# Calls within an attention head in another order on TensorE, ScalarE and VectorE

## The chip, the cores and the metric

The kernel runs on one core of one Trainium2 chip. The metric is the device time of one execution in microseconds (us). The kernel before takes a median of 836.47 us over 3 runs, between 835.2 and 836.91. TensorE (PE), VectorE (DVE), ScalarE (ACT) and GpSimd (POOL) each work through a queue of their own in program order; SyncE (SP) issues nearly all DMAs. They meet only through semaphores.

## What is computed

Attention in which a query sees only the keys of its own cluster, then two feed-forward layers, all in float32:

```python
# q, k, v: (2, 8, 768, 64); centroids: (8, 16, 64)
q_assign = argmax(q_n @ c_n.T); k_assign = argmax(k_n @ c_n.T)
scores = where(q_assign[:, None] == k_assign[None, :], q @ k.T / 8, -1e9)
attn = exp(scores - max(scores)); attn /= sum(attn) + 1e-9
x = reshape(attn @ v)                        # (1536, 512)
h = x @ w_in                                 # 512 -> 2048
x = where(h >= 1, h, where(h <= -1, 0, (h + 1) ** 2 / 4)) @ w_out
xn = x / rms(x) * rms_g
out = (silu(xn @ w_gate) * (xn @ w_val)) @ w_out2     # 512 -> 1536 -> 512
```

## The kernel before, in words

**The two stages.** Batch times heads gives 16 heads (`NH`), numbered 0 to 15. The attention of all heads fills roughly the first 286 us; the feed-forward layers follow, in 60 steps of products (`up`, L730, and `down`, L768). Every float32 operand is split in a high and a low part, so that a product is made of two or three products of parts. The first `up` waits for the last head's reciprocals (`reciprocals_copied`, L734).

**Blocks.** `blocks` (L291) calls a function `blk` of each engine for n = -3 to 16. Blocks -3 to 3 and 10 to 16 are written out (`fixed` is the number), blocks 4 to 9 are a loop over pairs of an even (u = 0) and an odd block (`fixed` is None). In block n the engines do, for four different heads at once:

- the probabilities and the output of head n ("pt"), with the last two output products of head n - 1;
- scores and exp of head n + 1, tiles 1 to 5, and tile 0 of head n + 2 (`scored`, L301);
- the mask of head n + 2 ("msk"), and the cluster products and the loading of q and k of head n + 3 ("asg", "t").

`on` and `present` leave out what lies outside heads 0 to 15. So block 14 has no loading, mask or cluster work, and block 16 only the end of head 15.

**The calls.** With the numbers that the prediction uses:

- `scores(t)` (PE, L585; called "scores t"): four products into the PSUM pair `ps_s`. There is one such pair, so it waits until `cut(t)` (DVE, L1317) of the tile before has read it. `cut` copies the tile to `sf` and takes its minimum; `exp(t)` (ACT, L869) makes probabilities in `pbuf` and their sum. `sf` has two buffers. Scores 5 begins a new head and waits for its q and k (`qk_assembled`).
- `probs_t(j)` (PE, L618, "probs j"), j = 0 to 8: four transposes of probabilities into one of four PSUM banks (`USES`, L242, gives each use its bank; `slot_free`, L265, waits for its last reader). `high(j)` (ACT, L861) and `low(j)` (DVE, L1327) split the bank into `pth` and `ptl`, three buffers each, and `pv(j)` (PE, L631, "pv j") multiplies these with the values `vs` into `ps_o`. Probs 0 of a head waits for all of its exps.
- `output` (ACT, L885) copies `ps_o` to `osb` after pv 8. SP moves half of it to the other partitions (`moved`, L510), POOL adds it (`tpair`, L2001).
- `transpose_qk` (PE, L648), `qk_high` (ACT, L897) and `qk_low` (DVE, L1361) load and split q and k; SP copies them in place (L496 to L499).
- `assign` (PE, L658), `assigned` and `hits` (DVE, L1369 and L1379), the rank product `eqr` (POOL, L2026), `masks` (DVE, L1346, two compares into `mskin`), `mask_t` (PE, L677, into `ps_o`, so it waits for `output`), `masks` (ACT, L907, into `stage`) and two SP copies (L513, L515) make a mask.
- `reciprocals` (DVE, L1336) inverts the sums, POOL widens them into `rsb` (L2017). In an even block from 2 on, `spread` (PE, L607) transposes `rsb` into `ps_s`, the same banks as the scores', `spread_out` (ACT, L880) copies it back, and scores 0 wait for that copy.
- POOL's block (L1970) is: the two `vs` calls for the next head, which wait until pv 8 of the head before has run; the output add; the final product `xr` (even) or the widening (odd); in blocks 1 to 3 and 10 to 15 preparations for the layers (`early`, L1941); then the rank product.
- `first_t` and `second_t` (ACT, DVE) split the first activations for the layers in blocks 11, 12 and 15.

**What sets the order.** In each `blk` the calls stand in one order written out by hand, the same for all blocks (PE L690 to L725, ACT L933 to L961, DVE L1399 to L1421). The orders on SP and POOL are written out too. The PE order at a block's start is spread, probs 1, scores 0, pv 7, q/k transposes, pv 8, scores 1.

## Time and profile before

| What | us |
|---|---|
| Median of 3 runs (lowest to highest) | 836.47 (835.2 to 836.91) |
| The profiled execution, its own time | 836.99 |
| Its span, first to last instruction | 835.2 |
| TensorE busy | 806.0 (97%) |
| VectorE busy | 646.2 (77%) |
| ScalarE busy | 492.9 (59%) |
| GpSimd busy | 403.3 (48%) |
| First product of the layers starts at | 286.21 |

The rows further down come from that one profiled execution, so their times are to be set against 836.99 us, which is the span and 1.8 us around it. TensorE's instructions are pipelined: a group's length runs until its last result is modelled as ready, and the next may start before that. The mean granted clock of TensorE is 0.994 of full speed.

### The profile page before, as it was taken

To read this page: it belongs to the slowest core of one execution; us is meant where nothing else is said; L and a number is where in the kernel's file an instruction comes from. 1 tells how busy PE (TensorE), PEld (TensorE's weight loads), DVE (VectorE), ACT (ScalarE), POOL (GpSimd) and SP (SyncE) were. 2 spreads that over 40 slices of the span, in tenths; PEclk is the share of its full clock that TensorE was granted. 3 is DMA by queue.
4 is the path that set the end of the run, shared out by engine and by line. 5 is a ranking of instruction groups with operands and counts; after the bars stand their busy time and mean duration, and the time that the engine had idled before them with its cause. 6 is when DMAs were issued, how large, how long until landed. Compare 5 with 4: busy or idle time off the path is not lost.

```text
span 835.2 us, 15332 instructions
## 1 busy us (share of the span) xinstructions
PE 806.0 (97%) x5357; PEld 732.9 (88%) x5357; DVE 646.2 (77%) x1219; ACT 492.9 (59%) x893; POOL 403.3 (48%) x355
## 2 busy tenths in 40 slices
PE   7999999999999899999999999999999999999998
PEld 5898898898888789999899999988988999999997
DVE  4898998899898787665666677997767787878666
ACT  3788887887887677665555558878333222222221
POOL 1034533344567890760660663896294472919000
PEclk8999999999999999999999999999999999999999
DMA  7866546655632000010110110210120201100012
GB/s 168 170 162 144 116 110 144 132 110 117 150 93 64 20 27 26 26 51 25 28 52 13 39 51 9 69 51 2 27 63 1 76 1 52 38 26 26 38 39 77
DMA packets 65507, 54.92 MB, mean 66 GB/s; under 512 B 30112, under 2 KB 52640, under 8 KB 65440
## 3 DMA queue, kind: packets, MB, share of 16 engines
q1 hardware_dynamic: 65264, 53.97, 26.2%
q8 instruction: 39, 0.64, 0.3%
q14 instruction: 28, 0.23, 0.1%
q10 hardware_dynamic: 176, 0.08, 0.0%
HBM read 27.30 MB, written 3.15 MB: 36 GB/s over the span
## 4 chain that ended last, share of the span: by engine, by line
PE 78%; DVE 8%; issue 6%; ACT 4%; POOL 3%; DMA 1%; DVEq 0%; SPq 0%; ACTq 0%; POOLq 0%
PE ps L763 34%; PE ps L785 14%; PE ps L797 11%; PE ps L643 5%; PE ps L600 4%; PE ps L627 4%; PE ps L603 3%; DVE ptl L1333 2%; DVE sf L1324 2%; POOL wl L1864 1%; ACT pbuf L877 1%; PE ps L671 1%; PE ps L672 1%; ACT rsb L883 1%; PE ps L574 1%
## 5 line engine op out<-in xcount | busy, mean ns | idle before, releaser
L763 PE MATMUL ps<-th,wh 128*128 128x256 f32 x840 | 239.2, 285 | 3.2 <-ACT snap L969 1.2
L763 PE MATMUL ps<-tl,wh 128*128 128x256 f32 x840 | 237.6, 283 | 0.0
L763 PE MATMUL ps<-th,wl 128*128 128x256 f32 x840 | 237.6, 283 | 0.0
L763 PEld LDWEIGHTS ps<-th,wh 128*128 128x128 f32 x840 | 160.9, 192 | 7.4 <-issue 1.6
L763 PEld LDWEIGHTS ps<-tl,wh 128*128 128x128 f32 x840 | 161.0, 192 | 2.0
L763 PEld LDWEIGHTS ps<-th,wl 128*128 128x128 f32 x840 | 160.9, 192 | 0.0
L1324 DVE TENSOR_SCALAR_CACHE_REDUCE sf<-ps 128x768 f32<-128x768 f32 x96 | 91.2, 951 | 29.0 <-PE ps L603 28.2
L1864 POOL TENSOR_TENSOR wl<-wraw,wh 128x448 fp32r<-128x448 f32 x80 | 106.6, 1361 | 1.3
L877 ACT ACTIVATE pbuf<-sf,minn 128x768 f32<-128x768 f32 x96 | 89.6, 934 | 21.0 <-DVE sf L1324 20.8
L867 ACT ACTIVATE pth<-ps 128x512 fp32r<-128x512 f32 x144 | 84.4, 589 | 29.2 <-PE ps L627 17.5
L1333 DVE TENSOR_TENSOR ptl<-ps,pth 128x512 fp32r<-128x512 f32 x144 | 95.5, 682 | 3.8 <-ACT pth L867 3.7
L1845 POOL TENSOR_TENSOR wraw<-corner,wraw 128x256 f32<-128x256 f32 x20 | 17.7, 886 | 150.9 <-DMA wraw<-in_moe_w_val 86.6
L1476 DVE TENSOR_TENSOR gl<-hid,gh 128x512 fp32r<-128x512 f32 x84 | 74.1, 887 | 16.5 <-ACT gh L999 15.1
L975 ACT ACTIVATE hid<-ps 128x256 f32<-128x256 f32 x60 | 22.8, 380 | 107.1 <-PE ps L763 106.9
L627 PE MATMUL ps<-ident,pbuf 128*128 128x128 f32 x576 | 85.1, 273 | 0.8 <-ACT pbuf L877 0.4
L999 ACT ACTIVATE gh<-hid 128x512 fp32r<-128x512 f32 x84 | 52.8, 628 | 43.0 <-DVE hid L1471 32.3
L627 PEld LDWEIGHTS ps<-ident,pbuf 128*128 128x128 f32 x576 | 68.8, 140 | 10.0 <-DVE ptl L1333 1.2
L1459 DVE TENSOR_TENSOR hid<-hid,curve 128x512 f32<-128x512 f32 x48 | 41.8, 871 | 45.6 <-ACT curve L990 45.6
L785 PE MATMUL ps<-gh,o1h 128*128 128x512 f32 x192 | 75.2, 392 | 0.7 <-DVE gl L1476 0.7
L785 PE MATMUL ps<-gl,o1h 128*128 128x512 f32 x192 | 75.0, 391 | 0.0
L785 PE MATMUL ps<-gh,o1l 128*128 128x512 f32 x192 | 74.7, 389 | 0.0
L600 PE MATMUL ps<-k,q 128*128 128x384 f32 x192 | 58.0, 384 | 11.5 <-DVE sf L1324 4.5
(141 smaller groups left out, 1794.2 us busy)
## 6 DMA issues: line engine op xcount, KB each, us to landing
q<-atile SPq DMA_DIRECT2D x32, 192.0 KB, 3.7
k<-atile SPq DMA_DIRECT2D x32, 192.0 KB, 3.6
o1raw<-in_moe_w_out SPq DMA_DIRECT2D x8, 512.0 KB, 3.8
nat<-in_q SPq DMA_DIRECT2D x16, 192.0 KB, 3.9
nat<-in_k SPq DMA_DIRECT2D x16, 192.0 KB, 4.0
q<-btile SPq DMA_DIRECT2D x16, 192.0 KB, 3.2
k<-btile SPq DMA_DIRECT2D x16, 192.0 KB, 4.0
vnat<-in_v SPq DMA_DIRECT2D x16, 192.0 KB, 3.7
```

What stands on the lines that cost most here:

```text
L600: pe.matmul(slot[:, j, 0:HALF], q1[:, s, ts * P:(ts + 1) * P], k1[:, s, j * HALF:(j + 1) * HALF], start=True, stop=False)
L627: last = pe.transpose(w[:, col + t * P:col + (t + 1) * P], pbuf[:, u, first + t, kt * P:(kt + 1) * P], ident[:, :])
L763: last = pe.matmul(dst[:, 0:HC], a[w][:, j, kt, :], b[c][:, j, kt, :], start=(opened and kt == 0 and i == 0), stop=(kt == KH - 1 and i == ...
L785: last = pe.matmul(bank(Y[m]), w[q % 2][:, e, o:o + P], x[b][:, e, :], start=(opens(s) and h == 0 and i == 0), stop=(closes(s) and h == 1 ...
L797: last = pe.matmul(bank(Y[m]), x[b][:, 0, m * P:(m + 1) * P], w[f][:, :], start=(opens(s) and i == 0), stop=(closes(s) and i == 2))
L867: act.activation(pth[:, j % 3], wbank(PT_AT[j]), ACT.Copy).then_inc(probs_high, 1)
L877: act.activation(pbuf[:, s, ts, :], sf[:, ts % 2, :], ACT.Exp, bias=minn[:, s, ts:ts + 1], scale=-1.0, accum_out=den[:, s, ts:ts + 1]).the ...
L999: act.activation(gh[s % 2][:, e, :], half_of(s, e), ACT.Copy).then_inc(hidden_high, 1)
L1324: dve.tensor_scalar(two(sf[:, ts % 2]), score_slot(fixed, t)[:, :, 0:HALF], MASKED, None, ALU.min, ALU.min, accum_out=minn[:, s, ts:ts + 1 ...
L1333: dve.tensor_tensor(ptl[:, j % 3], wbank(PT_AT[j]), pth[:, j % 3].bitcast(F32), ALU.subtract).then_inc(probs_low, 1)
L1476: dve.tensor_tensor(gl[s % 2][:, e, :], half_of(s, e), gh[s % 2][:, e, :].bitcast(F32), ALU.subtract).then_inc(hidden_low, 1)
L1864: pool.tensor_tensor(lo[:, o], raw[:, o], hi[:, o].bitcast(F32), ALU.subtract).then_inc(up_split, 1)
```

## The change

Within a block, the calls of PE, ACT and DVE come in another order. Even and odd blocks get orders of their own, and so do blocks -3, -2, -1, 14, 15 and 16; blocks 0 to 13 take the even or the odd one. `transpose_qk` tests by itself whether it has work, and the warm-up products move into `keep_busy`. The calls themselves, their waits, SP's and POOL's orders and the layers stay as they are.

```diff
--- before.py
+++ after.py
@@ -646,6 +646,8 @@
     last.then_inc(pv_done, 1)
 
 def transpose_qk(n, u, fixed):
+    if not on(fixed, "t"):
+        return
     for pos in (T_AT, T_AT + 1):
         slot_free(pe, n, fixed, pos)
     s = (u + 1) % 2
@@ -687,42 +689,144 @@
                          ident_r[:, :], start=True, stop=True)
     last.then_inc(mask_transposed, 1)
 
-def blk(n, u, fixed, pair):
-    before, after = (None if fixed is None else fixed + i for i in (-1, 1))
-    spread(n, u, fixed, pair)
-    probs_t(n, u, fixed, 1)
-    scores(n, u, fixed, pair, 0)
-    pv(n - 1, 1 - u, before, 7)
-    if on(fixed, "t"):
-        transpose_qk(n, u, fixed)
+def keep_busy(fixed):
     if fixed == -3:
         warm(2)
     elif fixed == -2:
         warm(4)
-    pv(n - 1, 1 - u, before, 8)
-    scores(n, u, fixed, pair, 1)
-    probs_t(n, u, fixed, 2)
-    mask_t(n, u, fixed)
-    probs_t(n, u, fixed, 3)
-    scores(n, u, fixed, pair, 2)
-    pv(n, u, fixed, 0)
-    pv(n, u, fixed, 1)
-    probs_t(n, u, fixed, 4)
-    pv(n, u, fixed, 2)
-    assign(n, u, fixed, range(0, NT // 2))
-    scores(n, u, fixed, pair, 3)
-    probs_t(n, u, fixed, 5)
-    pv(n, u, fixed, 3)
-    probs_t(n, u, fixed, 6)
-    scores(n, u, fixed, pair, 4)
-    assign(n, u, fixed, range(NT // 2, NT))
-    pv(n, u, fixed, 4)
-    pv(n, u, fixed, 5)
-    probs_t(n, u, fixed, 7)
-    scores(n, u, fixed, pair, 5)
-    probs_t(n, u, fixed, 8)
-    pv(n, u, fixed, 6)
-    probs_t(n + 1, 1 - u, after, 0)
+
+def blk(n, u, fixed, pair):
+    before, after = (None if fixed is None else fixed + i for i in (-1, 1))
+    if fixed == -3:
+        transpose_qk(n, u, fixed)
+        keep_busy(fixed)
+        assign(n, u, fixed, range(0, NT // 2))
+        assign(n, u, fixed, range(NT // 2, NT))
+    elif fixed == -2:
+        keep_busy(fixed)
+        transpose_qk(n, u, fixed)
+        mask_t(n, u, fixed)
+        assign(n, u, fixed, range(0, NT // 2))
+        assign(n, u, fixed, range(NT // 2, NT))
+        scores(n, u, fixed, pair, 5)
+    elif fixed == -1:
+        scores(n, u, fixed, pair, 0)
+        scores(n, u, fixed, pair, 1)
+        transpose_qk(n, u, fixed)
+        mask_t(n, u, fixed)
+        scores(n, u, fixed, pair, 2)
+        scores(n, u, fixed, pair, 3)
+        assign(n, u, fixed, range(0, NT // 2))
+        assign(n, u, fixed, range(NT // 2, NT))
+        scores(n, u, fixed, pair, 4)
+        scores(n, u, fixed, pair, 5)
+        probs_t(n + 1, 1 - u, after, 0)
+    elif fixed == NH - 2:
+        spread(n, u, fixed, pair)
+        pv(n - 1, 1 - u, before, 7)
+        pv(n - 1, 1 - u, before, 8)
+        scores(n, u, fixed, pair, 0)
+        probs_t(n, u, fixed, 1)
+        probs_t(n, u, fixed, 2)
+        pv(n, u, fixed, 0)
+        scores(n, u, fixed, pair, 1)
+        probs_t(n, u, fixed, 3)
+        probs_t(n, u, fixed, 4)
+        pv(n, u, fixed, 1)
+        scores(n, u, fixed, pair, 2)
+        pv(n, u, fixed, 2)
+        pv(n, u, fixed, 3)
+        probs_t(n, u, fixed, 5)
+        scores(n, u, fixed, pair, 3)
+        probs_t(n, u, fixed, 6)
+        probs_t(n, u, fixed, 7)
+        pv(n, u, fixed, 4)
+        scores(n, u, fixed, pair, 4)
+        pv(n, u, fixed, 5)
+        probs_t(n, u, fixed, 8)
+        pv(n, u, fixed, 6)
+        probs_t(n + 1, 1 - u, after, 0)
+    elif fixed == NH - 1:
+        pv(n - 1, 1 - u, before, 7)
+        pv(n - 1, 1 - u, before, 8)
+        probs_t(n, u, fixed, 1)
+        probs_t(n, u, fixed, 2)
+        pv(n, u, fixed, 0)
+        probs_t(n, u, fixed, 3)
+        pv(n, u, fixed, 1)
+        probs_t(n, u, fixed, 4)
+        probs_t(n, u, fixed, 5)
+        pv(n, u, fixed, 2)
+        probs_t(n, u, fixed, 6)
+        pv(n, u, fixed, 3)
+        probs_t(n, u, fixed, 7)
+        pv(n, u, fixed, 4)
+        probs_t(n, u, fixed, 8)
+        pv(n, u, fixed, 5)
+        pv(n, u, fixed, 6)
+    elif fixed == NH:
+        spread(n, u, fixed, pair)
+        pv(n - 1, 1 - u, before, 7)
+        pv(n - 1, 1 - u, before, 8)
+    elif u == 0:
+        spread(n, u, fixed, pair)
+        pv(n - 1, 1 - u, before, 7)
+        pv(n - 1, 1 - u, before, 8)
+        scores(n, u, fixed, pair, 0)
+        probs_t(n, u, fixed, 1)
+        transpose_qk(n, u, fixed)
+        mask_t(n, u, fixed)
+        scores(n, u, fixed, pair, 1)
+        probs_t(n, u, fixed, 2)
+        pv(n, u, fixed, 0)
+        probs_t(n, u, fixed, 3)
+        pv(n, u, fixed, 1)
+        scores(n, u, fixed, pair, 2)
+        probs_t(n, u, fixed, 4)
+        pv(n, u, fixed, 2)
+        probs_t(n, u, fixed, 5)
+        scores(n, u, fixed, pair, 3)
+        assign(n, u, fixed, range(0, NT // 2))
+        assign(n, u, fixed, range(NT // 2, NT))
+        pv(n, u, fixed, 3)
+        scores(n, u, fixed, pair, 4)
+        probs_t(n, u, fixed, 6)
+        pv(n, u, fixed, 4)
+        probs_t(n, u, fixed, 7)
+        scores(n, u, fixed, pair, 5)
+        probs_t(n, u, fixed, 8)
+        pv(n, u, fixed, 5)
+        pv(n, u, fixed, 6)
+        probs_t(n + 1, 1 - u, after, 0)
+    else:
+        scores(n, u, fixed, pair, 0)
+        pv(n - 1, 1 - u, before, 7)
+        pv(n - 1, 1 - u, before, 8)
+        probs_t(n, u, fixed, 1)
+        transpose_qk(n, u, fixed)
+        mask_t(n, u, fixed)
+        scores(n, u, fixed, pair, 1)
+        probs_t(n, u, fixed, 2)
+        probs_t(n, u, fixed, 3)
+        pv(n, u, fixed, 0)
+        scores(n, u, fixed, pair, 2)
+        pv(n, u, fixed, 1)
+        probs_t(n, u, fixed, 4)
+        assign(n, u, fixed, range(0, NT // 2))
+        probs_t(n, u, fixed, 5)
+        scores(n, u, fixed, pair, 3)
+        pv(n, u, fixed, 2)
+        pv(n, u, fixed, 3)
+        probs_t(n, u, fixed, 6)
+        assign(n, u, fixed, range(NT // 2, NT))
+        scores(n, u, fixed, pair, 4)
+        pv(n, u, fixed, 4)
+        probs_t(n, u, fixed, 7)
+        pv(n, u, fixed, 5)
+        scores(n, u, fixed, pair, 5)
+        probs_t(n, u, fixed, 8)
+        probs_t(n + 1, 1 - u, after, 0)
+        pv(n, u, fixed, 6)
 
 blocks(pe, blk)
 
@@ -930,35 +1034,102 @@
         if fixed == NH - 1:
             second_t_hi(first, count)
 
-    spread_out()
-    high(0)
-    high(1)
-    exp(0)
-    output()
-    qk_high()
-    masks()
-    high(2)
-    exp(1)
-    high(3)
-    first_t(0)
-    exp(2)
-    high(4)
-    first_t(4)
-    second_t(0, 1)
-    high(5)
-    first_t(1)
-    second_t(1, 1)
-    exp(3)
-    high(6)
-    first_t(5)
-    first_t(2)
-    exp(4)
-    high(7)
-    first_t(6)
-    first_t(3)
-    high(8)
-    second_t(2, 2)
-    exp(5)
+    if fixed == -3:
+        qk_high()
+    elif fixed == -2:
+        qk_high()
+        masks()
+        exp(5)
+    elif fixed == -1:
+        qk_high()
+        masks()
+        exp(0)
+        exp(1)
+        exp(2)
+        exp(3)
+        exp(4)
+        exp(5)
+    elif fixed == NH - 2:
+        spread_out()
+        high(0)
+        output()
+        high(1)
+        high(2)
+        exp(0)
+        high(3)
+        exp(1)
+        high(4)
+        high(5)
+        exp(2)
+        high(6)
+        high(7)
+        exp(3)
+        high(8)
+        exp(4)
+    elif fixed == NH - 1:
+        second_t(0, 1)
+        high(0)
+        output()
+        high(1)
+        second_t(1, 1)
+        high(2)
+        high(3)
+        high(4)
+        high(5)
+        high(6)
+        high(7)
+        high(8)
+        second_t(2, 1)
+        second_t(3, 1)
+    elif fixed == NH:
+        spread_out()
+        output()
+    elif u == 0:
+        spread_out()
+        first_t(4)
+        output()
+        high(0)
+        high(1)
+        masks()
+        qk_high()
+        high(2)
+        exp(0)
+        high(3)
+        high(4)
+        exp(1)
+        exp(2)
+        high(5)
+        first_t(5)
+        exp(3)
+        high(6)
+        exp(4)
+        first_t(6)
+        high(7)
+        high(8)
+        exp(5)
+    else:
+        first_t(0)
+        high(0)
+        output()
+        high(1)
+        masks()
+        qk_high()
+        high(2)
+        first_t(1)
+        exp(0)
+        high(3)
+        exp(1)
+        high(4)
+        exp(2)
+        high(5)
+        first_t(2)
+        first_t(3)
+        high(6)
+        exp(3)
+        exp(4)
+        high(7)
+        high(8)
+        exp(5)
 
 blocks(act, blk)
 
@@ -1396,29 +1567,102 @@
         if fixed == NH - 1:
             second_t_lo(first, count)
 
-    cut(0)
-    low(0)
-    masks()
-    low(1)
-    cut(1)
-    qk_low()
-    low(2)
-    cut(2)
-    low(3)
-    reciprocals()
-    cut(3)
-    low(4)
-    low(5)
-    second_t(0, 1)
-    cut(4)
-    assigned()
-    low(6)
-    second_t(1, 1)
-    hits()
-    cut(5)
-    low(7)
-    low(8)
-    second_t(2, 2)
+    if fixed == -3:
+        qk_low()
+        assigned()
+        hits()
+    elif fixed == -2:
+        masks()
+        qk_low()
+        assigned()
+        hits()
+        cut(5)
+    elif fixed == -1:
+        cut(0)
+        masks()
+        cut(1)
+        qk_low()
+        cut(2)
+        cut(3)
+        assigned()
+        cut(4)
+        hits()
+        cut(5)
+    elif fixed == NH - 2:
+        reciprocals()
+        low(0)
+        cut(0)
+        low(1)
+        cut(1)
+        low(2)
+        low(3)
+        cut(2)
+        low(4)
+        cut(3)
+        low(5)
+        low(6)
+        cut(4)
+        low(7)
+        low(8)
+    elif fixed == NH - 1:
+        reciprocals()
+        low(0)
+        low(1)
+        low(2)
+        low(3)
+        low(4)
+        low(5)
+        low(6)
+        low(7)
+        low(8)
+        second_t(0, 1)
+        second_t(1, 1)
+        second_t(2, 1)
+        second_t(3, 1)
+    elif fixed == NH:
+        pass
+    elif u == 0:
+        reciprocals()
+        masks()
+        cut(0)
+        low(0)
+        low(1)
+        cut(1)
+        qk_low()
+        low(2)
+        cut(2)
+        low(3)
+        low(4)
+        cut(3)
+        low(5)
+        assigned()
+        cut(4)
+        hits()
+        low(6)
+        cut(5)
+        low(7)
+        low(8)
+    else:
+        masks()
+        cut(0)
+        low(0)
+        low(1)
+        cut(1)
+        reciprocals()
+        qk_low()
+        low(2)
+        cut(2)
+        low(3)
+        cut(3)
+        low(4)
+        low(5)
+        assigned()
+        cut(4)
+        low(6)
+        hits()
+        cut(5)
+        low(7)
+        low(8)
 
 blocks(dve, blk)
 
```

## Rows read from the trace of the kernel before

**Rows 1.** Stretches: length, busy PE, PEld, DVE, ACT, POOL; then TensorE clock, DMA.
```profile
286.21:835.20 548.99, 540.48 (x3564) 495.75 (x3564) 402.99 (x705) 270.45 (x483) 280.70 (x230) 1.00 0.12 36
129.01:161.74 32.73, 31.42 (x222) 28.64 (x223) 28.89 (x60) 26.78 (x50) 10.81 (x11) 1.00 0.57 126
194.48:227.69 33.21, 31.84 (x222) 28.70 (x222) 30.60 (x60) 28.22 (x54) 19.50 (x18) 1.00 0.57 125
227.69:259.33 31.64, 29.84 (x204) 26.63 (x204) 27.39 (x56) 27.48 (x52) 19.05 (x17) 1.00 0.37 90
259.33:286.21 26.88, 23.22 (x145) 19.00 (x145) 21.83 (x36) 18.48 (x36) 21.47 (x20) 1.00 0.13 35
31.23:46.56 15.33, 14.71 (x104) 13.18 (x103) 13.22 (x30) 12.85 (x24) 1.82 (x3) 1.00 0.90 209
```

**Rows 2.** TensorE in order of time, an odd block: start, length, what, idle before.
```profile
147.72 0.60 PE L627 MATMUL ps<-ident,pbuf 128*128 128x128 f32 x4
148.47 0.54 PE L686 MATMUL ps<-ident_r,mskin 128*32 128x128 f32 x6 [0.15 <-ACT osb L891]
148.85 0.62 PE L627 MATMUL ps<-ident,pbuf 128*128 128x128 f32 x4
149.69 0.62 PE L600 MATMUL ps<-k,q 128*128 128x384 f32 x2 [0.21 <-DVE sf L1324]
...
154.08 0.47 PE L643 MATMUL ps<-pth,vs 128*128 128x512 f32 x1
...
154.62 0.60 PE L627 MATMUL ps<-ident,pbuf 128*128 128x128 f32 x4
154.97 0.60 PE L600 MATMUL ps<-k,q 128*128 128x384 f32 x2
...
155.76 0.20 PE L671 MATMUL ps<-cb,atile 128*128 x1
...
159.85 0.87 PE L614 MATMUL ps<-ident,rsb 128*128 128x128 f32 x6
160.56 0.60 PE L627 MATMUL ps<-ident,pbuf 128*128 128x128 f32 x4
161.74 0.62 PE L600 MATMUL ps<-k,q 128*128 128x384 f32 x2 [0.58 <-ACT rsb L883]
```

**Rows 3.** ScalarE in order of time, the same boundary between blocks.
```profile
160.90 0.79 ACT L883 ACTIVATE rsb<-ps 128x768 f32<-128x768 f32 x1
```

**Rows 4.** Groups of VectorE and ScalarE, 129.01 to 161.74 us: busy, mean ns, idle.
```profile
L1333 DVE TENSOR_TENSOR ptl<-ps,pth 128x512 fp32r<-128x512 f32 x18 | 11.9, 682 | 0.0
L1324 DVE TENSOR_SCALAR_CACHE_REDUCE sf<-ps 128x768 f32<-128x768 f32 x12 | 11.4, 951 | 3.6 <-PE ps L603 3.4
...
L877 ACT ACTIVATE pbuf<-sf,minn 128x768 f32<-128x768 f32 x12 | 11.2, 934 | 2.0 <-DVE sf L1324 2.0
```

**Rows 5.** All engines by time in block 13, and VectorE's mask compares (`mskin`).
```profile
245.96 1.00 POOL L1983 TENSOR_TENSOR vs<-vnat,vs 128x384 fp32r<-128x384 f32 x1
...
246.13 1.12 DVE L1356 TENSOR_TENSOR mskin<-ramp,m 128x96 fp32r<-128x96 f32 x2
...
247.39 0.52 PE L686 MATMUL ps<-ident_r,mskin 128*32 128x128 f32 x6 [0.69 <-DVE mskin L1356]
...
L1356 DVE TENSOR_TENSOR mskin<-ramp,m x32: 245/255/948, 11.8 to 247.0; 128x96 fp32r<-128x96 f32 x32
```

**Rows 6.** TensorE in order of time, block -2: the mask transposes.
```profile
12.75 0.84 PE L686 MATMUL ps<-ident_r,mskin 128*32 128x128 f32 x6
```

**Rows 7.** POOL by time, blocks 14 and 15, and the moved half's transfers.
```profile
261.44 0.51 POOL L1980 TENSOR_SCALAR vs<-vnat 128x384 fp32r<-128x384 f32 x1 [4.69 <-issue]
...
276.19 1.06 POOL L1875 TENSOR_SCALAR o1h<-o1raw 128x1024 fp32r<-128x1024 f32 x1
279.75 1.82 POOL L2001 TENSOR_TENSOR tpair<-osb,moved 64x768 f32<-64x768 f32 x1 [2.50 <-issue]
...
DMA to landing us min/median/max: 2.5/2.6/3.8
```

## The prediction

> **What bounds the kernel now.** I read the windows view first. After 286.21 us TensorE is busy for 540.48 of 548.99 us, and the change touches nothing there. What it can move lies before: a regular pair of heads takes 32.73 us, pair 10-11 takes 33.21, pair 12-13 takes 31.64, and 26.88 us pass from the first scores of block 14 to the first product of the expert layers [rows 1]. In a regular pair TensorE is busy 31.42 us, VectorE 28.89 and ScalarE 26.78 [rows 1].
>
> The busy time hides what a wait costs, so I next read TensorE's instructions in order of time and took starts, not lengths. Where nothing is waited for, pv 3 takes the slot from 154.08 to 154.62 us (0.54), four transposes of probabilities the one to 154.97 (0.35, though their last result is ready only after 0.60), and a scores tile the one to 155.76 (0.79) [rows 2]. With those slots the odd block of the pair shows three losses:
> - The mask transposes start 0.40 us late (147.72 + 0.35 = 148.07, they start at 148.47, released by ScalarE's output copy) [rows 2].
> - Scores 1 start 0.49 us late (148.85 + 0.35 = 149.20, start 149.69, released by VectorE's cut) [rows 2].
> - After the spreading of reciprocals, scores 0 of the next block start 0.83 us late (160.56 + 0.35 = 160.91, start 161.74): they need the bank that ScalarE's copy of `rsb` empties, 160.90 to 161.69 [rows 2, 3].
>
> The even block repeats the first two; the trace has both twice in each pair. A pair so loses 0.83 + 2 x 0.40 + 2 x 0.49 = 2.61 us, and TensorE's own slots fill 32.73 - 2.61 = 30.1 us. VectorE needs 28.89, so it can follow, but without room: it is the second limit, at 96% of the first.
>
> **The change, regular pairs.** No instruction is added or removed; the cost is in who waits for whom. T is the start of the spread in an even block.
>
> *Even block.* The spread (slot 0.71, from 159.85 to 160.56 [rows 2]) is now followed by pv 7 and 8 (0.54 each at most), so scores 0 are asked for at about T+1.75. Their bank is free once ScalarE has done exp 5 (0.93, [rows 4]), which starts with the spread since both wait for cut 5, and the copy (0.79, [rows 3]): T+1.72. The 0.83 loss closes. Pv 7 and 8 end at T+1.95, so the output copy ends at T+2.8, and the mask transposes, now behind scores 0 (to T+2.55), probs 1 (T+2.9) and the q/k transposes (T+3.5), find it done. Cut 0 stands behind low 8 (to T+1.3), the reciprocals (T+1.7) and masks (T+2.9 with the wait for scores 0 in it) and ends at T+3.9, when scores 1 are asked for. I walked the rest call by call, with 0.60 for a low and 0.88 for a cut from start to start (their means are 0.682 and 0.951, each overlaps its successor [rows 4]). VectorE ends cut 1, 2, 3, 4 at T+6.0, 8.4, 10.5, 12.95; TensorE asks for scores 2, 3, 4, 5 at T+6.5, 8.6, 11.05, 13.05. QK_low ends at T+6.9, before probs 4 want its banks at T+7.3. Nothing is late by over 0.1. The odd block starts at T+15.55.
>
> *Odd block.* Scores 0 come first, pv 7 and 8 find their lows, the masks are made before cut 0, and mask transposes wait 0.05. One stall is left, scores 3 on cut 2 (0.2), because qk_low stands before it behind the reciprocals. Scores 5 at T+28.5 give cut 5 at T+30.5, when the next spread is asked for. So a pair takes 30.5 us, 2.25 less.
>
> *The queues that stay.* SP's and POOL's calls keep their order. SP's mask copies are issued at about T+4.9 in the even block and needed by scores 5 at T+13; the output half moves earlier too. I cost both at nothing; if that cover went, the wait would come before scores 5.
>
> *A new price: VectorE beside POOL.* The earlier end of pv 8 also starts POOL's two `vs` calls earlier, at T+2.0 to T+3.6, just where VectorE now makes the masks. In block 13 of before the two mask compares ran beside such a call: they took 1.12 us together and ended at 247.25, behind POOL's call that ended at 246.96, and TensorE idled 0.69 [rows 5]. The median of one compare is 0.255, so two are 0.5. Per even block the price lies between nothing and 1.0, the length of the second `vs` call. I take 0.5, because the compares and the call start within half a microsecond of each other and either may come first. A regular pair gains 2.25 - 0.5 = 1.75; four of them (heads 2 to 9) give 7.0.
>
> **The other stages.**
> - *Pair 10-11.* POOL has 19.50 us of work there instead of 10.81 [rows 1]. Its rank product comes after weights and sums, by the walk at T+17.4, and the odd block's VectorE queue now *starts* with masks(), wanted at T+16.4. Cut 0 and low 0 are queued behind. 1.0 is lost: gain 1.0, after 0.25 from losses this pair had beyond the regular ones.
> - *Pair 12-13.* Block 13 adds the 0.69 idle of [rows 5] to the regular losses. Gain 1.75 + 0.45 = 2.2.
> - *Blocks 0 and 1.* From scores to scores block 0 takes 15.33 [rows 1]. It has neither a spread nor pv calls of a head before, its slots add to 13.7, and the walk gives 13.8; I take 1.2 of the 1.5, because its DMA queues are the fullest (share 0.90 in that window). Block 1 goes from scores 0 to scores 0 of a block with a spread; the walk gives 0.2.
> - *Blocks -3 to -1.* Block -2's four warm-up products move ahead of the q/k transposes, into the time in which these wait; the mask transposes then follow at once instead of at 12.75 [rows 6]. That may bring the mask copies forward by up to 0.8. Against it, in block -1 ScalarE's exp 0 now waits behind the copy of q/k and masks, up to 0.5 later for head 0's last exp. Bounds: 0.8 gained to 0.5 lost; I take 0.3 gained.
> - *Blocks 14 to 16.* POOL sets the end: from `vs` at 261.44 it is busy without a wait until `o1h` ends at 277.25, 15.8 us; then it waits 2.50 us for the moved half of head 14's output, adds at 279.75, widens the last reciprocals, makes the first sum, and behind that sum's rounding and the `rsb` copy on ScalarE the first product starts at 286.21: 6.46 us after the add [rows 7]. Here `vs` may start at T+2.0, when pv 8 of head 13 ends, so POOL is free at T+17.9. Block 14's PE calls have no q/k, mask or assignment work, and the walk ends head 14's output copy at T+15.8. Its transfer takes 2.5 to 3.8 us [rows 7] and 0.2 to issue, so the add starts between T+18.5 and T+19.9, and the first product between T+25.0 and T+26.4. Counted from scores 0 of block 14 (T+1.75) that is 23.2 to 24.6 against 26.88 [rows 1]: gain 2.3 to 3.6; I take 2.9, the middle. What is late next is the same add, on the transfer.
>
> **The sum.** 0.3 + 1.2 + 0.2 + 7.0 + 1.0 + 2.2 + 2.9 = 14.8 us. The profiled execution took 836.99 us (span 835.2 and 1.8 around it); 836.99 - 14.8 = 822.2. The median of before, 836.47, lies 0.5 below it, so I forecast 821.7. With all upper values (0.8, 1.5, 0.2, 9.0, 1.5, 2.8, 3.6: 19.4) it would be 817.1.
>
> **Rivals.**
> 1. *The lock bites whole.* VectorE's mask compares, which read two tensors in SBUF, stand behind the whole second `vs` call in every even block. For: block 13's row. Against: in the other blocks the four compares cost little. Price: 1.0 instead of 0.5 in seven even blocks, 3.5 us: 825.2. Chance 0.14. The Trainium skill, page SBUF — State Buffer, section Who interferes with whom, says that a VectorE instruction with two SBUF inputs contends with a GpSimd instruction reading SBUF, and that whoever comes first keeps the port; by that rule, this rival. The trace agrees in block 13 (1.12 us instead of about 0.5).
> 2. *VectorE becomes the bound.* It idled 3.84 us a pair. If in-order waits on highs and scores leave 3.0 of that, a pair takes 31.9 and gains 0.85, not 1.75: six pairs keep 5.4 and the tail 0.9 less, 828.0. For: 28.89 of work for 30.1. Against: three buffers of pth and ptl let a late low pass. Chance 0.10.
> 3. *Slower: the head of the odd VectorE queue.* masks() waits there for POOL's rank product, with cut 0, hence scores 1, behind it. If POOL is held by the moved half or by VectorE's port, each microsecond beyond T+16.4 is a microsecond of the pair. It decides from 2.5 us late in each of six pairs, which eats the whole 14.8; at 3.0 late (18 us) the time is 839.7. Before, the product followed the hits at once in a regular pair, which speaks against. Chance 0.05.
> 4. *No effect.* TensorE's starts would be bound by its own instruction rate, and each closed wait reappears as slower slots. The 0.35 slots beside waits speak against. 836.5, chance 0.02.
> 5. *More than the upper values* (below 817): 0.05.
>
> **How the numbers follow.** The forecast has 0.64, within 817 to 826. The range goes from 816.5, the upper values with a little more, to 829, which takes in rivals 1 and 2; outside are most of 3, 4 and half of 5. A measurement here can tell 0.2%, 1.7 us, from no change. Faster than that: 0.64 + 0.14 + 0.10 + 0.05 = 0.93; same 0.02; slower 0.05.
>
> **What would show it.** In the pair stage scores 0 after the spread start without idle time on the `rsb` copy; the mask transposes no longer wait for the output copy; a pair takes 30.5 to 31.3 us. VectorE's compares of even blocks last 0.5 to 1.5 us beside the second `vs`. In pair 10-11 VectorE idles on the rank product. The first product of the layers starts near 271.5 us. The forecast is wrong if a pair stays over 32 us, if scores wait for cuts in a new place for over 0.5 a head, or if the stage after it is not as long as before (549.0 us).

## The result, and the profile after

The changed kernel takes a median of 826.94 us (825.69, 825.97, 827.92, 827.95) against 836.69 for the kernel before (835.20 to 838.02 in 4 runs). The ratio is 0.9883, with a 95% interval from 0.9859 to 0.9908: about 1.2% faster. The profiled execution took 827.92 us (span 826.1).

The windows view, with the stretches cut at the same instructions as in [rows 1] (columns: length, busy time and instructions of PE, PEld, DVE, ACT and POOL, TensorE's granted clock, DMA share, GB/s):

```profile
274.27:826.10 551.83, 541.91 (x3564) 495.84 (x3564) 406.73 (x707) 270.01 (x483) 279.03 (x230) 1.00 0.12 36
126.89:157.88 30.99, 30.99 (x223) 28.44 (x222) 28.23 (x61) 26.29 (x49) 10.71 (x11) 1.00 0.59 133
188.91:221.18 32.27, 30.96 (x224) 28.41 (x223) 28.76 (x61) 28.49 (x54) 19.38 (x18) 1.00 0.57 129
221.18:251.10 29.92, 29.00 (x205) 26.35 (x204) 26.86 (x55) 27.02 (x52) 18.89 (x17) 1.00 0.42 100
251.10:274.27 23.17, 21.25 (x143) 18.14 (x143) 18.69 (x32) 18.95 (x36) 20.84 (x20) 1.00 0.14 41
31.79:48.13 16.34, 16.34 (x104) 15.47 (x103) 13.65 (x28) 11.44 (x23) 1.56 (x2) 0.84 0.82 190
```

Line by line against [rows 1]: the layers take 551.83 us instead of 548.99, a regular pair 30.99 instead of 32.73 (and TensorE is busy for all of it), pair 10-11 32.27 instead of 33.21, pair 12-13 29.92 instead of 31.64, the end of the attention 23.17 instead of 26.88. Block 0 got longer, 16.34 instead of 15.33, and its granted clock is 0.84.

Counted from the start of one spread to the next, which takes in all blocks, the two profiled executions differ like this:

| Stretch | Forecast gain | Gain |
|---|---|---|
| Blocks -3 to -1 (to scores 0 of block 0) | 0.3 | -0.56 |
| Block 0 | 1.2 | -1.01 |
| Block 1, to the first spread (61.78, now 63.04) | 0.2 | 0.31 |
| Four regular pairs (to 192.67, now 187.10) | 7.0 | 6.83 |
| Pair 10-11 (to 225.97, now 219.43) | 1.0 | 0.97 |
| Pair 12-13 (to 257.61, now 249.38) | 2.2 | 1.69 |
| Blocks 14 to 16 (to 286.21, now 274.27) | 2.9 | 3.71 |
| Layers | 0 | -2.84 |
| Sum | 14.8 | 9.10 |

**The pair.** TensorE by time, then ScalarE, VectorE and POOL, at a boundary that answers to [rows 2, 3] (start, length, what, idle before):

```profile
125.00 0.87 PE L614 MATMUL ps<-ident,rsb 128*128 128x128 f32 x6
...
126.20 0.50 PE L643 MATMUL ps<-pth,vs 128*128 128x512 f32 x1
...
126.89 0.62 PE L600 MATMUL ps<-k,q 128*128 128x384 f32 x2
...
128.71 0.61 PE L688 MATMUL ps<-ident_r,mskin 128*32 128x128 f32 x6
129.16 0.57 PE L600 MATMUL ps<-k,q 128*128 128x384 f32 x2
...
126.05 0.79 ACT L987 ACTIVATE rsb<-ps 128x768 f32<-128x768 f32 x1
...
126.83 0.43 DVE L1527 TENSOR_TENSOR mskin<-ramp,m 128x96 fp32r<-128x96 f32 x2
...
127.13 0.52 POOL L2224 TENSOR_SCALAR vs<-vnat 128x384 fp32r<-128x384 f32 x1 [2.45 <-PE ps L643]
127.73 1.01 POOL L2227 TENSOR_TENSOR vs<-vnat,vs 128x384 fp32r<-128x384 f32 x1
```

Spread, pv 7, pv 8 and scores 0 follow each other without idle time; the `rsb` copy (126.05 to 126.84) is done when scores 0 start at T+1.89. The mask transposes and scores 1 wait for nothing. All three losses of [rows 2] are gone. The weight loads of scores 0 still wait for the copy, which ends at T+1.84:

```profile
126.89 0.30 PEld L600 LDWEIGHTS ps<-k,q 128*128 128x128 f32 x2 [0.40 <-ACT rsb L987]
```

So pv 7 and 8 cover the copy with nothing to spare. The two mask compares take 0.43 us, no more than twice the median of one in [rows 5]: they start 0.30 us ahead of POOL's first `vs` call.

**Pair 10-11.** VectorE and TensorE at the start of block 11:

```profile
205.09 0.35 DVE L1521 TENSOR_REDUCE m<-eqr 128x12 f32<-128x192 f32 x1 [1.49 <-POOL eqr L2270]
205.48 1.25 DVE L1527 TENSOR_TENSOR mskin<-ramp,m 128x96 fp32r<-128x96 f32 x2
...
206.87 0.52 PE L688 MATMUL ps<-ident_r,mskin 128*32 128x128 f32 x6 [1.04 <-DVE mskin L1527]
207.66 0.62 PE L600 MATMUL ps<-k,q 128*128 128x384 f32 x2 [0.27 <-DVE sf L1495]
```

VectorE waits 1.49 us for POOL's rank product; its compares then run beside a `vs` call and take 1.25 us for the two. TensorE loses 1.04 + 0.27.

**The end of the attention and the layers.** POOL and VectorE around head 14's output add and the first product, then VectorE's split product `gl` and POOL's `wh`, both in step 22 of the layers:

```profile
268.44 1.83 POOL L2245 TENSOR_TENSOR tpair<-osb,moved 64x768 f32<-64x768 f32 x1 [1.25 <-issue]
...
273.17 1.82 DVE L1484 TENSOR_TENSOR tl<-xr,th 128x512 fp32r<-128x512 f32 x2
274.91 1.23 DVE L1484 TENSOR_TENSOR tl<-traw,th 128x512 fp32r<-128x512 f32 x1
276.06 1.51 DVE L1484 TENSOR_TENSOR tl<-xr,th 128x256 fp32r<-128x256 f32 x1
277.49 0.41 DVE L1672 TENSOR_TENSOR pair<-ps,snap 128x256 f32<-128x256 f32 x1
...
517.30 2.11 DVE L1720 TENSOR_TENSOR gl<-hid,gh 128x512 fp32r<-128x512 f32 x1
...
517.18 1.69 POOL L2099 TENSOR_SCALAR wh<-wraw 128x1792 fp32r<-128x1792 f32 x1
```

The add starts at T+19.06 (T = 249.38), against 279.75 in [rows 7], and the first product at T+24.89. Behind it the splits of block 15 keep VectorE to 277.49, 3.22 us after the first product; before, that sum started 1.73 us after it. The first step is 0.76 us longer for it. In steps 22 to 24, where `gl` takes 2.11 instead of its median of 0.69 us, the layers fall back by another 2.9 us, of which 0.9 return later. The rest of the -2.84, 0.1, is spread thinly.

### The profile page after: what moved, and what is told of

Same layout as the page of the kernel before. It is cut to its first block and busy times, and to the rows that moved or that the text cites. A ratio compares the mean times of both kernels' runs of the same rounds, so it can differ in the third digit from the quotient of the medians.

```text
span 826.1 us, 15344 instructions
## 1 busy us (share of the span) xinstructions
PE 805.7 (98%) x5357; PEld 735.1 (89%) x5357; DVE 642.2 (78%) x1219; ACT 490.3 (59%) x893; POOL 400.3 (48%) x355
## 5 line engine op out<-in xcount | busy, mean ns | idle before, releaser
L1720 DVE TENSOR_TENSOR gl<-hid,gh 128x512 fp32r<-128x512 f32 x84 | 73.8, 884 | 16.5 <-ACT gh L1170 15.1
L643 PE MATMUL ps<-pth,vs 128*128 128x512 f32 x192 | 64.7, 378 | 0.7 <-DVE ptl L1504 0.5
```

Of the source, the lines that this page charges most:

```text
L643: last = pe.matmul(ps_o[:, t0 // 4, 0:count * P], vs[:, u, kt, :], part[:, j % 3, col:col + count * P], start=(kt == 0 and i == 0), stop=( ...
L1720: dve.tensor_tensor(gl[s % 2][:, e, :], half_of(s, e), gh[s % 2][:, e, :].bitcast(F32), ALU.subtract).then_inc(hidden_low, 1)
```

## The experiments

Unless said otherwise each kernel is the changed one with one edit. Spread times are the starts in the profiled execution, and a pair is the distance between two of them.

**1. The old order of a block's start.**

```diff
                     spread(n, u, fixed, pair)
-                    pv(n - 1, 1 - u, before, 7)
-                    pv(n - 1, 1 - u, before, 8)
-                    scores(n, u, fixed, pair, 0)
                     probs_t(n, u, fixed, 1)
+                    scores(n, u, fixed, pair, 0)
+                    pv(n - 1, 1 - u, before, 7)
+                    pv(n - 1, 1 - u, before, 8)
                     transpose_qk(n, u, fixed)
```

> The changed kernel with probs 1 and scores 0 ahead of pv 7 and 8 again in the even blocks 0 to 12 of TensorE. Theory A (the 0.83 us a pair came back because pv 7 and 8 cover ScalarE's copy of rsb): scores 0 wait for the copy again by 0.5 to 0.8 us, a pair takes 31.5 to 31.9 instead of 31.0, time 3 to 5 us longer, 830 to 832. Rival B (the pairs are bound by VectorE, which has 28.9 of work): a pair stays at 31.0 to 31.2.

Measured: 829.52 us (828.55 to 829.86; ratio 0.9920 [0.9900, 0.9941]). Regular pairs take 32.11 to 32.27 us instead of 30.90 to 31.11. TensorE in this kernel:

```profile
127.05 0.60 PE L627 MATMUL ps<-ident,pbuf 128*128 128x128 f32 x4
128.23 0.62 PE L600 MATMUL ps<-k,q 128*128 128x384 f32 x2 [0.58 <-ACT rsb L987]
```

The wait on the `rsb` copy is back with the same 0.58 us as in [rows 2], and behind it the mask transposes wait 0.41 us for the output copy. Together with what follows this costs 1.1 to 1.2 us a regular pair, more than theory A's 0.5 to 0.8. The two pv calls are what covers the copy, and rival B falls: with VectorE as the bound the pairs would have stayed near 31.1. The whole time is only 2.6 us above the changed kernel's, less than was expected, because the layers of this profile last 548.73 us and not 551.83 (experiment 4 has the reason).

**2. Parts of the change alone.** The first kernel has the orders of before in blocks -3 to -1, the second also in blocks 14 to 16, so that only blocks 0 to 13 are new.

```diff
+                if fixed is not None and fixed < 0:
+                    ... (the orders of before, on PE, ACT and DVE)
+                    return
```

> The changed kernel with the first three blocks (-3 to -1) back in the old orders on TensorE, ScalarE and VectorE. Where the changed kernel starts scores 0 of block 2's spread at 63.04 us, before did at 61.78, although blocks 0 and 1 were forecast to give 1.4. Theory A (the new orders of the first blocks cost it, by leaving TensorE idle or late so that its clock is granted at half rate longer, 9.6 to 23 and 31 to 37 us instead of 12 to 24 us): the first spread comes at 60 to 61.5 us and the time falls by 1.5 to 3 us, to 824 to 825.5. Rival B (blocks 0 and 1 in the new order cost it): the first spread stays near 63 and the time at 827.

> New orders in blocks 0 to 13 alone; blocks -3 to -1 and 14 to 16 have those of before. If the gains add as the walk has them, the spreads up to block 14 start as in the kernel with the old first blocks (61.4 to 61.8, then every 30.8 to 31.1 us, block 14's near 248), the last two gaps are those of before, 25.7 and 2.9 us, so that the first product comes near 276.5 us, and the layers last 548.4 to 549, without the 0.76 us in their first step: 825 to 827 us in the better runs, some 3 us above the kernel with old first blocks alone. Rival (the tail was paced by GpSimd alone, and the earlier vs call would bring most of the gain with the old orders too): the last gaps are 23 to 24 us and the time is that of the changed kernel.

Measured, first kernel: 825.13 us (823.40, 823.53, 826.72, 829.65; ratio 0.9884 [0.9845, 0.9923]), first spread at 61.38. That start is what theory A asked for, but it decides nothing: the unedited changed kernel has its first spread at 61.56 in its second profile (experiment 4). Second kernel: 826.71 us (824.67 to 828.02; ratio 0.9884 [0.9864, 0.9904]). Its last two gaps are 25.08 and 2.88 us; with the new orders they were 22.72 and 2.22 in another run of the changed kernel. So the new orders of blocks 14 to 16 bring the first product 3.02 us forward. The layers of the second kernel last 547.89 us, and their first step is not longer: VectorE there starts the first sum 1.73 us after the first product. Part of the tail's gain is therefore paid back in the layers. The rival in which POOL alone paces the tail falls.

**3. The splits of block 15 back between the lows.**

```diff
                     low(5)
+                    second_t(0, 1)
                     low(6)
+                    second_t(1, 1)
                     low(7)
                     low(8)
-                    second_t(0, 1)
-                    second_t(1, 1)
```

> The changed kernel with VectorE's first two splits for the layers (second_t 0 and 1) back between low 5, 6 and 7 of block 15, as before. In the changed kernel they stand behind low 8 and run at 273.2 to 275 us, the third and fourth until 277.6, and the first step's sums start at 277.5. Theory A (they delay the first step by 0.76 us): the first down products start 10.6 us after the first up product, as before, instead of 11.3, and the time falls by up to 0.8. Rival B (the splits late in block 15 then delay lows and with them pv: the first product comes later by as much): no change in time.

Measured: 827.16 us (823.77 to 827.63; ratio 0.9893 [0.9872, 0.9913]). The first step of the layers is short again, but the first product comes 2.86 us after the last spread instead of 2.13. POOL and TensorE show why:

```profile
268.90 1.29 POOL L2261 TENSOR_SCALAR rsb<-rec 128x768 f32<-128x768 f32 x1 [0.18 <-PE ps L627]
270.16 1.71 POOL L2169 TENSOR_TENSOR traw<-xr 128x512 f32<-128x512 f32 x1
...
273.59 0.39 PE L867 MATMUL ps<-th,wh 128*128 128x256 f32 x1 [0.87 <-ACT rsb L987]
```

VectorE's splits at 268.82 and 270.02 now run beside POOL's widening and first sum, which take 1.29 and 1.71 us; in the changed kernel they take 0.83 and 1.29. ScalarE waits for that sum, TensorE for ScalarE. What the first step gains is lost ahead of the first product: the 0.76 us is moved, not removed. The profiled run is the fastest of the four; what the other three, at 827.14 to 827.63 us, did in the layers was not seen.

**4. POOL held at step 22.** POOL makes one of its weight preparations of the layers only after VectorE's first `gl` of that step.

```diff
+            pool.wait_ge(hidden_low, HALVES[22] + 1)
             high_up(9)
```

> The changed kernel with one wait more on POOL: the rounding of the tenth up weights (high_up 9) waits until VectorE has made the low part of step 22. In the changed kernel's profile that low part took 2.11 us at 517.3 beside POOL's rounding (0.73 before), and six half-steps of the layers from there on lose 2.4 us that before does not lose. Theory A (VectorE and POOL meet at the port there, by the phase at which the weights land): the loss of 2.4 us goes or falls under 1, time 824.5 to 826. Rival B (the phase shifts the meeting to the next calls, or the loss has another cause): the stage from the first product on stays at 551 to 552 us, time 827, or worse by the wait.

> The changed kernel itself once more, beside the others of this call. Theory A (the layers' loss of the profiled run, 551.83 us instead of 549, comes and goes from run to run as GpSimd's preparations fall beside VectorE's gl products): the times fall in two groups, near 824 to 826 and near 827 to 828, and if this profile belongs to the first its layers last 549 to 550 us. Theory B (the loss belongs to the new orders): the layers last 551.5 to 552 us again, the median is 827 us and no run is below 825.5.

Measured: held 824.64 us (823.21 to 825.67; ratio 0.9858 [0.9834, 0.9882]), layers 549.71. The changed kernel again, on another chip: 827.14 us (826.82 to 827.67; ratio 0.9887 [0.9868, 0.9906]), layers 551.97. The eight runs of the changed kernel lie between 825.69 and 827.95, the four with POOL held all below them, though by only 0.02 us at the nearest and on other chips. `wh` and `gl` at the same place, one pair of rows each for the old first blocks of experiment 2, the changed kernel again, and POOL held (POOL row, DVE row):

```profile
515.75 2.23 POOL L2190 TENSOR_SCALAR wh<-wraw 128x1792 fp32r<-128x1792 f32 x1
515.73 0.68 DVE L1811 TENSOR_TENSOR gl<-hid,gh 128x512 fp32r<-128x512 f32 x1
```

```profile
516.34 1.69 POOL L2099 TENSOR_SCALAR wh<-wraw 128x1792 fp32r<-128x1792 f32 x1
...
516.46 2.10 DVE L1720 TENSOR_TENSOR gl<-hid,gh 128x512 fp32r<-128x512 f32 x1
```

```profile
517.30 1.71 POOL L2099 TENSOR_SCALAR wh<-wraw 128x1792 fp32r<-128x1792 f32 x1 [0.64 <-DVE gl L1720]
...
516.19 1.02 DVE L1720 TENSOR_TENSOR gl<-hid,gh 128x512 fp32r<-128x512 f32 x1
```

The order of two starts that are 0.02 to 0.12 us apart decides. With POOL first by 0.12, `gl` takes 2.10; with VectorE first by 0.02, `gl` takes 0.68 and POOL's copy stretches from 1.69 to 2.23. In the three profiles where POOL was first (both of the changed kernel and experiment 5) the layers last 551.41 to 551.97 us; in the ten other profiles of these experiments 547.89 to 549.71.

A stretched `gl` does not cost by itself. The kernel before and the ten other kernels have one too, later, in step 23 (1.98 to 2.00 us). In the first kernel of experiment 2 it is this one (POOL row, DVE row), and TensorE has no idle time over 0.1 us between 512 and 544 us:

```profile
529.86 1.70 POOL L2190 TENSOR_SCALAR wh<-wraw 128x1792 fp32r<-128x1792 f32 x1
530.12 1.99 DVE L1811 TENSOR_TENSOR gl<-hid,gh 128x512 fp32r<-128x512 f32 x1 [0.37 <-ACT gh L1236]
```

In the three profiles with the early meeting TensorE does wait behind it, in the first 0.64 us at 520.39 and 0.39 us at 536.16.

Theory B's signs all came in the second set of runs: layers of 551.97 us, a median of 827.14 and no run below 825.5. Theory A is not ruled out by them. The first four runs of the changed kernel do fall into two groups, 825.69 and 825.97 against 827.92 and 827.95, and only one of the slower two was profiled; the faster two may have missed the meeting, which no trace shows. Nor is the meeting bound to the new orders of the pairs alone, for the kernels of experiments 2 and 3 have those and missed it in their profiles. What the rows show is a matter of phase: POOL has waited some 7 us for weights that a DMA brings, and the moment at which it comes back decides beside which `gl` its copy falls. The kernel before had its `wh` 11 us later, at 528.63.

The Trainium skill, page SBUF — State Buffer, section Who interferes with whom, says that a VectorE instruction with two SBUF inputs contends with a GpSimd instruction that reads SBUF, and that the order of issue decides who blocks. The trace agrees, and the blocking is whole to 0.2 us: POOL's 1.69 us from 517.18 end at 518.87, and `gl` ends 0.54 us later, at 519.41, where it takes 0.68 by itself.

**5. The rank product first.** In block 10 POOL makes the second of two sums behind the rank product.

```diff
                 if fixed == NH - 6:
                     fill_out(0)
                     t_sum(0, 0, 1)
-                    t_sum(0, 1, 1)
...
                                        ALU.mult).then_inc(assignment_ranked, 1)
+                if fixed == NH - 6:
+                    t_sum(0, 1, 1)
```

> The changed kernel, but in block 10 GpSimd makes the second of its two sums (1.31 us) behind the rank product instead of ahead of it. If the 1.0 us price of pair 10-11 is the odd VectorE queue waiting at its head for the rank product, the pair falls from 32.33 to 31.0 to 31.4 us, VectorE's wait for it from 1.5 us to 0.3 or less, and the first product comes 1.0 us earlier. Rival (the pair is long because GpSimd's 19.50 us beside VectorE slow the splits down): the wait goes and the pair stays above 32 us. The whole time would show 1 us less at best.

Measured: 825.62 us (823.75 to 826.62; ratio 0.9863 [0.9841, 0.9886]), pair 10-11 31.88 us instead of 32.56 in the changed kernel run beside it. VectorE at the start of block 11:

```profile
203.26 0.35 DVE L1521 TENSOR_REDUCE m<-eqr 128x12 f32<-128x192 f32 x1 [0.32 <-POOL eqr L2269]
203.65 1.41 DVE L1527 TENSOR_TENSOR mskin<-ramp,m 128x96 fp32r<-128x96 f32 x2
```

The wait went from 1.5 to 0.3 us, as the first theory had it, but the pair kept half of its excess: the compares now run beside the sum that was moved (203.19 to 204.47) and take 1.41 us, and TensorE still loses 0.4 us on them and 0.3 on the cut behind. Both theories had a part of it. In the five later profiles with this edit the pair takes 31.22, 31.31, 31.94 and 31.25 us in four and 32.48 in one, where the compares hold TensorE up for 1.19 us. Without the edit it takes 32.33 to 32.86 in six profiles and 31.93 in the kernel of experiment 1. So the edit is worth 0.4 to 1.6 us in most profiles and nothing in one; the compares beside POOL are what varies.

**6. The parts put together.** Old first blocks, rank product first and POOL held; then, later and side by side on another chip, the same without the old first blocks, that one with 14 more warm-up products, and the full combination again.

```diff
                     assign(n, u, fixed, range(NT // 2, NT))
+                    warm(14)
                     scores(n, u, fixed, pair, 5)
                 elif fixed == -1:
```

> Old orders in blocks -3 to -1, the rank product ahead of the second sum in block 10, and GpSimd held at half-step 22 so that its later preparations come behind VectorE's product. If the three add: first spread 61.4 to 61.8, pair 10-11 near 31.2, first product near 271.7, layers 548.9 to 549.8, no run above 825: a median of 822.5 to 823.5 us, below the changed kernel by 2 to 4 us. If they do not, the median is that of the kernel with GpSimd held, 824.6.

> The changed kernel with its own first blocks, the rank product first in block 10, and GpSimd held at half-step 22. If the first blocks' orders give nothing either way (their difference is TensorE's granted clock and the DMAs, which vary from run to run), this is within 0.8 us of the combination with the old first blocks (823.2): 822.5 to 824.5. If the new orders of blocks -3 to -1 cost about 1 us, it is 824.3 or more and the same kernel with old first blocks is 1 us lower in this call too.

> The combination of old first blocks, rank product first and GpSimd held, once more beside the two: 823 to 824 us again. It differs from the first kernel of this call in blocks -3 to -1 alone. Spreads every 30.7 to 31.2 us from 60.6 to 62.6 on, layers 548.9 to 549.8, no gl product of 2 us near 516 us.

> As the kernel before it in this call, with 14 more warm-up products on TensorE where it idles 3.2 us ahead of the first scores (block -2). Idea: TensorE's granted clock is 0.50 from some 15 to 23 us and often again from 29 to 36 us, in block 0, behind idle stretches; with the 3.2 us filled, the clock is 1.00 when the first scores start. Then scores 0 to 1 of block -1 run at 0.64 each instead of 1.28, block 0 takes 14.2 us instead of 15.6 to 16.3, and the first spread comes near 60.5: 1 to 2 us less, a median of 821.5 to 823. Rival (the DMAs of q and k set the start, so p0 stays at 30.2 to 31.5 and only the clock changes): less than 0.5 us between the two medians. A third case: the lower clock comes all the same, and the products push the first scores back by up to 1 us.

| Kernel | Median us (range, runs) | Ratio to before |
|---|---|---|
| Combination | 823.24 (821.81 to 824.54, 5) | 0.9837 [0.9818, 0.9856] |
| Later: without old first blocks | 825.20 (822.92 to 825.82, 6) | 0.9837 [0.9809, 0.9865] |
| Later: that with more warm-up | 827.68 (824.55 to 829.31, 6) | 0.9868 [0.9837, 0.9898] |
| Later: combination again | 822.67 (822.04 to 825.36, 6) | 0.9819 [0.9790, 0.9848] |

The combination beats both kernels: 1.6 to 1.8% under the one before, and 3.9 us under the changed kernel run beside it (827.14). In the later runs the kernel with the new orders of blocks -3 to -1 is 2.5 us slower in the medians, though the two ranges overlap. Five of the six runs of the combination lie at or below 823.50; five of the six without old first blocks lie at 824.60 or above. The granted clock over the whole execution differs too: 0.988 to 0.992 in the six without old first blocks, 0.991 to 0.996 in five of the six of the combination. The two runs at 0.991, one of each kernel, took 822.92 and 823.50 us. So much of the 2.5 us may be the clock, and whether the orders bring the lower clock or it came by chance is not shown.

The warm-up products did the opposite of what was meant. TensorE in that kernel, and the windows of its clock (length, busy time and instructions, granted clock, DMA share, GB/s):

```profile
17.75 4.83 PE L574 MATMUL ps<-ones 128*128 128x512 f32 x14
22.42 0.51 PE L600 MATMUL ps<-k,q 128*128 128x384 f32 x2
```

```profile
17.00:24.00 7.00, 6.99 (x29) 0.76 1.05 229
...
24.00:31.00 7.00, 6.41 (x42) 1.00 0.49 90
31.00:38.00 7.00, 5.96 (x29) 0.52 0.89 200
```

They ran partly at half clock, took 4.83 us and held the first scores back to 22.42 (18.0 to 19.2 in all others). The clock was 1.00 from 24 to 31 us, with TensorE busy for 6.41 of these 7, and yet 0.52 in the 7 behind them. The third case came true, and by more than its 1 us: the first scores came 3 to 4 us later, and the median is 2.5 us above that of the kernel without these products.

**7. One call of the first blocks moved back.** The kernel without old first blocks of the table above, with ScalarE's exp 0 of block -1 first again.

```diff
                 elif fixed == -1:
+                    exp(0)
                     qk_high()
                     masks()
-                    exp(0)
                     exp(1)
```

> As the kernel with new first blocks, the rank product first and GpSimd held (825.20 us), with one call moved back: in block -1 ScalarE does exp 0 ahead of the copy of q/k and the masks, as before the change. In the profile of that kernel exp 0 stands from 26.18 us behind those two, which wait 1.82 us for TensorE's transposes; with the old first blocks it ran at 22.37. Theory A (this one move is what the new first blocks cost): head 0's probabilities are transposed 11.5 to 12.0 us after the first scores instead of 12.5 to 12.7, near 30.4 us, the first spread comes at 60.2 to 61.6 where TensorE's clock stays at 1.00 in block 0, and the median falls to 822.5 to 823.8, that of the kernel with old first blocks (822.67). Theory B (it is the warm-up products ahead of the transposes in block -2, or TensorE's clock alone): the distance stays at 12.5 to 12.7 us and the median at 824.6 to 825.8.

Measured: 823.60 us (821.24 to 826.02, 4 runs; ratio 0.9857 [0.9837, 0.9877]), by itself on another chip. ScalarE by time in block -1, without the edit and with it:

```profile
24.69 0.90 ACT L1008 ACTIVATE atile<-ps,fold 128x768 fp32r<-128x768 f32 x1 [1.82 <-PE ps L657]
25.49 0.78 ACT L1016 ACTIVATE stage<-ps 32x768 fp32r<-32x768 f32 x1
26.18 0.92 ACT L981 ACTIVATE pbuf<-sf,minn 128x768 f32<-128x768 f32 x1
```

```profile
22.14 0.94 ACT L981 ACTIVATE pbuf<-sf,minn 128x768 f32<-128x768 f32 x1 [0.25 <-DVE sf L1495]
...
23.84 0.91 ACT L1008 ACTIVATE atile<-ps,fold 128x768 fp32r<-128x768 f32 x1 [0.68 <-PE ps L657]
```

Exp 0 runs 4 us earlier, in time in which ScalarE had waited 1.82 us. The median and the first spread (60.15, with a clock of 1.00 in block 0) are what theory A asked for. But the distance from the first scores to head 0's first probabilities is 12.30 us, between what theory A (11.5 to 12.0) and theory B (12.5 to 12.7) asked for, and by its ratio to before the kernel is no better than without the edit. That distance is a poor sign besides: it is 11.48 to 12.24 us in the four profiles of experiments with old first blocks and 11.91 to 12.73 in the seven with new ones, so the two ranges overlap. Which edit in blocks -3 to -1 costs is left open.

**The clock in the first blocks.** The profiles differ most there. The windows of block 0 in the changed kernel's second profile and in the combination's second, to be set against 16.34 us at 0.84 above:

```profile
31.88:46.14 14.26, 14.15 (x106) 13.20 (x104) 13.77 (x29) 11.68 (x23) 1.82 (x3) 1.00 0.92 218
```

```profile
31.05:45.27 14.22, 14.10 (x102) 13.19 (x103) 13.76 (x29) 11.67 (x23) 1.84 (x3) 1.00 0.90 214
```

At a granted clock of 1.00 (2.4 GHz) throughout, block 0 takes 14.2 to 14.3 us, with new or old first blocks (five profiles); where a stretch of 0.50 (1.2 GHz) falls into it, 14.4 to 16.5 (eight).

## Why the prediction was right or wrong

The forecast was 821.7 us with a range from 816.5 to 829.0; 826.94 lies in the range, 5.2 us above the forecast. By its profile the change gained 9.1 us where 14.8 were summed. Step by step:

- **Regular pairs: right.** 6.83 of 7.0 us. The three losses read off TensorE's starts went, and experiment 1 shows the largest by itself. Two errors nearly cancelled. The lock's price of 0.5 us a pair was not paid, since the compares start ahead of `vs` (by 0.30 us in the rows shown) and take 0.25 to 0.26 us each in all blocks of the regular pairs, so rival 1 did not happen and the sign of 0.5 to 1.5 us beside the second `vs` did not come. And the walk's 30.5 us was 0.5 too short: scores 0 start at T+1.89 for T+1.75, since ScalarE's copy of `rsb` ends at T+1.84 for T+1.72, and TensorE, now busy without a gap, fills 31.0 us; the slots that "fill 30.1 us" were a little longer in the crowd. Where the rest of it lies was not tried. VectorE did not become the bound (rival 2).
- **Pair 10-11: right, with its mechanism.** 0.97 of 1.0. The head of the odd VectorE queue waits 1.49 us for the rank product, and experiment 5 takes that wait away. What was not in the sum is VectorE's compares beside POOL, on which 0.7 are still lost once the wait is gone.
- **Pair 12-13:** 1.69 of 2.2; two waits of 0.46 each are left there, one of pv on a low and one of the mask transposes on the output copy.
- **Blocks 14 to 16: the term was too small.** 3.71 instead of 2.9, above the bound of 3.6. The add starts at T+19.06, inside the bounds, but the end behind it took 5.83 us, not the 6.46 of [rows 7] that the sum carried over, as if the reordering left it alone.
- **Blocks -3 to 0: wrong, in sign.** The sum had 1.5 us, the profile shows -1.57. Block 0's term was right at full clock: 15.33 - 14.26 = 1.07 of 1.2. The step that failed is that the clock was taken as in the profile before, where block 0 ran at 1.00; in 8 of the 13 profiles with its new order a stretch at 0.50 reaches into it. For blocks -3 to -1 the sum had 0.3 gained, which the runs do not bear out. The profile shows 0.56 lost, and experiment 6 has 2.5 us more in the medians with a lower clock. Over all profiles the loss is smaller than the scatter: scores 0 of block 0 start at 30.93 to 32.48 us (31.74 in the mean of seven) with the new orders and at 31.05 to 32.00 (31.57 in the mean of four) with the old. Head 0's last exp does come later, as its bound had it, but by 0.8 us in the mean where the bound was 0.5: it starts 11.35 us behind the first scores with the new orders, 10.57 with the old (five profiles, the one of before among them). The wait of 1.1 to 2.0 us for TensorE's q/k transposes, which now stands ahead of exp 0, was not seen.
- **The layers: wrong.** "The change touches nothing there" is true of the code and not of the time. 0.76 us follow VectorE's splits, which the new order of block 15 puts behind all lows; POOL sums beside them stretch them. This was in the diff, and the forecast looked only up to the first product. Another 2.0 in the profiled run come from a meeting of `gl` and `wh` 243 us later, decided by a tenth of a microsecond. That could not have been worked out from the trace of before; that the layers' time might change at all with POOL's phase could have been a rival, and it was not.

The sign named at the end of the forecast, "if the stage after it is not as long as before (549.0 us)", was the one that struck, and the first product came at 274.27 instead of near 271.5. That the time still lies in the range owes something to the width of the range, 12.5 us: the stages before the layers gained 11.9 of 14.8 us, and the layers took 2.8 of it back.

## What to carry to other kernels

Walking the starts call by call, with slots from stretches that wait for nothing, forecast a steady pair here to 0.5 us of 31; it says nothing of stages at either end, so give the first blocks' clock and the stage behind the change terms and bounds of their own. When a reordering shifts a stage in time, look in the next stage for pairs of two-input VectorE and POOL instructions that start together, and let the one that nobody waits for go second: one wait of POOL went with 2.3 to 2.5 us here, more than the 1.7 of a reordered pair. Trust a profile of one run for what it shows, and not for how often it happens. Work moved out of a full stage is only gained if it does not land ahead of the next stage's first sum.

## What the runs showed of the hardware

- Two instructions 0.12 us apart: POOL's copy first (1.69 us) and VectorE's product takes 2.11 instead of 0.69; VectorE first by 0.02 and it takes 0.68, POOL's copy 2.23. A `gl` of 1.99 us in step 23 left TensorE without idle time, one of 2.11 in step 22 went with waits of 0.64 and 0.39 us.
- TensorE's granted clock in the first 37 us differs between executions of the same program: the changed kernel's two profiles have it at 0.51 and at 1.00 from 30 to 37 us. Filling an idle stretch with 14 products did not keep it up. What decides it, these runs do not show.
